# Requesting residual rows one tile earlier, splitting the last product of the second layer, and moving two copies at the layer change

## The reference

```python
# attention: q pooled in pairs, out = softmax(q_pool @ k.T / 8) @ v
x = attn_out.transpose(0, 2, 1, 3).reshape(1152, 512)
# layer m=0: top-1 routing, each expert takes at most cap tokens
e = argmax(x @ w_gate); g = softmax(x @ w_gate)[e]
out[i] = g[i] * (relu(x[i] @ w1[e]) @ w2[e])      # kept tokens, else 0
# layer m=1: tokens with x @ w_skip > 0 are routed without a limit
do = x @ w_skip > 0
out = x.copy()
out[do] = x[do] + g * (relu(x[do] @ w1b[e]) @ w2b[e])
```

## Time and profile before

| | |
|---|---|
| median of 3 runs | 615.25 us (614.92 to 615.62) |
| the profiled execution, its own time | 616.29 us |
| its span, first to last instruction | 614.5 us |
| outside the span | 1.8 us |
| PE busy | 591.7 us (96%) |
| DVE, ACT, POOL busy | 313.5 (51%), 266.3 (43%), 188.5 us (31%) |
| mean granted clock of PE | 0.992 of full speed |

### The profile page before, as it was taken

The page is one execution under the profiler, slowest core; times in us unless marked ns, Lnnn a source line. Parts: engine busy times, 40 slices in busy tenths (PEclk is TensorE's granted clock), DMA queues, the critical chain, the costliest instruction groups (busy, mean ns, idle before and its releaser), DMA issues.

```text
span 614.5 us, 12427 instructions
## 1 busy us (share of the span) xinstructions
PE 591.7 (96%) x3711; PEld 351.9 (57%) x3712; DVE 313.5 (51%) x659; ACT 266.3 (43%) x438; POOL 188.5 (31%) x164
## 2 busy tenths in 40 slices
PE   8899999999999999999999999999899999999992
PEld 7677787777777777777333333333594333333330
DVE  5457565757575766656353963955665220322220
ACT  4655565555565655620344444442102444444410
POOL 4785535444352800001011121122212122222222
PEclk9999999999999999999999999999989999999997
DMA  8979818171621062004999697762757789831111
GB/s 205 291 185 257 185 40 170 43 161 50 145 47 38 3 221 107 22 11 138 402 404 362 256 391 274 260 272 64 272 186 253 265 306 330 318 135 44 45 52 55
DMA packets 42637, 111.61 MB, mean 182 GB/s; under 512 B 16020, under 2 KB 16020, under 8 KB 41536
## 3 DMA queue, kind: packets, MB, share of 16 engines
q1 hardware_dynamic: 38528, 99.03, 50.8%
q0 software_dynamic: 4080, 12.22, 5.7%
HBM read 102.68 MB, written 12.06 MB: 187 GB/s over the span
## 4 chain that ended last, share of the span: by engine, by line
PE 88%; DVE 3%; issue 3%; DMA 2%; ACT 2%; POOLq 0%; DVEq 0%; POOL 0%; SPq 0%; ACTq 0%
PE psum L932 40%; PE psum L701 14%; PE psum L715 12%; PE psum L749 9%; PE psum L919 4%; PE psum L782 3%; PE psum L840 2%; PE psum L761 1%; PE psum L745 1%; DVE probs L1204 1%; ACT probs L1045 1%; PE psum L934 1%; DMA qraw<-in_q_dram 1%; DMA res<-moe_in,idx_r 1%; DMA xraw<-moe_in,rows_in 1%
## 5 line engine op out<-in xcount | busy, mean ns | idle before, releaser
L932 PE MATMUL psum<-w1ring,XT 128*64 x304 | 134.5, 595 | 0.8 <-issue 0.3
L932 PE MATMUL psum<-w2ring,HT 128*64 x320 | 133.7, 571 | 1.3 <-DVE wright L318 0.7
L934 PE MATMUL psum<-wright,XT 128*64 128x512 f32 x304 | 134.5, 595 | 0.0
L934 PE MATMUL psum<-wright,HT 128*64 128x512 f32 (+1 forms) x320 | 133.7, 571 | 0.0
L1204 DVE TENSOR_SCALAR_CACHE_REDUCE probs<-psum 128x1152 f32<-128x1152 f32 x72 | 97.6, 1357 | 62.5 <-PE psum L701 62.5
L1045 ACT ACTIVATE probs<-probs,nmax 128x1152 f32<-128x1152 f32 x72 | 90.7, 1260 | 45.6 <-DVE probs L1204 45.6
L701 PE MATMUL psum<-KT,QT 128*128 128x384 f32 x480 | 102.0, 350 | 2.7 <-DVE probs L1204 1.8
L932 PEld LDWEIGHTS psum<-w2ring,HT 128*64 128x64 f32 x320 | 43.7, 137 | 85.0 <-issue 83.0
L701 PEld LDWEIGHTS psum<-KT,QT 128*128 128x128 f32 x480 | 80.2, 188 | 14.7 <-issue 7.9
L932 PEld LDWEIGHTS psum<-w1ring,XT 128*64 128x64 f32 x304 | 40.1, 137 | 79.7 <-issue 79.7
L715 PE MATMUL psum<-ident,probs 128*128 128x128 f32 x648 | 82.0, 275 | 1.1 <-ACT probs L1045 0.6
(11 more groups left out here) (164 smaller groups left out, 636.7 us busy)
## 6 DMA issues: line engine op xcount, KB each, us to landing
w1ring<-in_moe_w_dram SPq DMA_DIRECT2D x64, 512.0 KB, 7.1
w2ring<-in_moe_w_dram SPq DMA_DIRECT2D x64, 512.0 KB, 7.4
qraw<-in_q_dram SPq DMA_DIRECT2D x30, 288.0 KB, 10.1
kraw<-in_k_dram SPq DMA_DIRECT2D x14, 576.0 KB, 9.0
V<-in_v_dram SPq DMA_DIRECT2D x8, 576.0 KB, 3.9
moe_in<-zero SPq DMA_DIRECT2D x9, 256.0 KB, 3.1
wnext<-in_next_w_dram SPq DMA_DIRECT2D x1, 2304.0 KB, 17.2
out_dram<-moe_in SPq DMA_DIRECT2D x1, 2304.0 KB, 9.4
```

The costliest lines, as they stand in the source:

```text
L932: pe.matmul(psum[0:GRAIN, b, 0:width], lhs[:, c * P:c * P + GRAIN], left, start=first, stop=last, skip_group_check=True)
L934: return pe.matmul(psum[GRAIN:P, b, 0:width], lhs[:, c * P + GRAIN:(c + 1) * P], wright[k][:, cols], start=first, stop=last, skip_group_ch ...
```

## The change

On POOL the order of requests in `step(t)` changes, and in layer 1 the residual rows are those of tile t instead of t-1. Before: residual rows of tile t-1, x of tile t+2, store of y of tile t-1. Now: residual rows of tile t, store of y of tile t-1, x of tile t+2. In layer 0, which has no residual, the store now stands ahead of x. Behind the loop, layer 1 no longer requests residual rows; it waits for a new semaphore `orow_half` and stores.

On PE the last y product of layer 1 also goes through `last_y_product`, in two halves; DVE adds the residual to each half by itself. The two copies of `yT` at the end of layer 0 move from DVE to ACT. DVE's wait with a value from a table becomes a wait for the constant 1 on a semaphore of its own, `last_logits`. PE reads the expert of the first tile ahead of `turn_x(0)` instead of behind it, and `keep_busy` between the counts and `r_ids` issues 13 products instead of 14, in both layers.

```diff
@@ -197,7 +197,8 @@
-        ylast_copied, y_half = sem("ylast_copied"), sem("y_half")
+        ylast_copied, last_logits = sem("ylast_copied"), sem("last_logits")
+        y_half_, orow_half = [sem(f"y_half_{m}") for m in range(2)], sem("orow_half")
...
@@ -633,18 +634,16 @@
                 def count_before(t):
 
                     if isinstance(t, int):
-                        return {0: 0, 1: 0, 2: 1 + m}[t]
-                    return t * (2 + m) - (3 + m)
-
-                def after(t, n):
-                    return count_before(t) + 1 + n
+                        return {0: 0, 1: m, 2: 1 + 2 * m}[t]
+                    return t * (2 + m) - 3
 
                 def step(t, first=False):
-                    if m == 1 and not first:
-                        load_residual(t - 1, after(t, 0))
-                    load_x(t + 2, after(t, 0 if first else m))
+                    count = count_before(t)
+                    if m == 1:
+                        load_residual(t, count + 1)
                     if not first:
-                        store_y(t - 1, after(t, m if isinstance(t, int) else m + 1))
+                        store_y(t - 1, count + (1 + m))
+                    load_x(t + 2, count + (2 + m))
 
                 n = ROUTED[m]
                 token = token_id if m == 0 else slot_token
@@ -667,13 +666,13 @@
                 with pool.Fori(2, NSLOT) as t:
                     with pool.If(t < rest + 2):
                         step(t)
-                done = rest * (2 + m) + (1 + m)
+                done = rest * (2 + m) + (1 + 2 * m)
                 if m == 0:
                     store_y(rest + 1, done + 1, last=True)
                     pool.wait_ge(y_stored, rest * 16 + 32)
                 else:
-                    load_residual(rest + 1, done + 1)
-                    store_y(rest + 1, done + 2)
+                    pool.wait_ge(orow_half, 1)
+                    store_y(rest + 1, done + 1)
                 pool.wait_ge(x_loaded, rest * 16 + 64)
                 settle()
 
@@ -884,7 +883,7 @@
                     for t in range(n):
                         mm = counted(whole, t, t + 1, n + 1)
                 mm.then_inc(pos_ready, 1)
-                keep_busy((14, 14)[m], HID_BANK + 1)
+                keep_busy((13, 13)[m], HID_BANK + 1)
 
                 pe.wait_ge(ids_ready, m + 1)
                 for t in range(n):
@@ -934,10 +933,14 @@
                     return pe.matmul(psum[GRAIN:P, b, 0:width], lhs[:, c * P + GRAIN:(c + 1) * P], wright[k][:, cols],
                                      start=first, stop=last, skip_group_check=True)
 
-                def hidden_product(t):
+                def hidden_place(t):
 
                     expert = left_expert(t)
-                    slot = pe.snap(ring_slot(FIRST, m, expert))
+                    return expert, pe.snap(ring_slot(FIRST, m, expert))
+
+                def hidden_product(t, place=None):
+
+                    expert, slot = place or hidden_place(t)
                     wait(pe, relu_ready, t)
                     for c in range(DC):
                         pe.wait_ge(w_loaded[FIRST][c], expert * 16 + (E * m + 1) * 16)
@@ -980,7 +983,7 @@
                             at = c * DM + half * 2 * P
                             mm = product(SECOND, HT, (Y_BANK, X_BANK)[half], c, slice(at, at + 2 * P), slot,
                                          c == 0, c == FC - 1, 2 * P)
-                        mm.then_inc((y_half, y_done)[half], 1)
+                        mm.then_inc((y_half_[m], y_done)[half], 1)
 
                 def turn_hidden(t):
                     pe.wait_ge(relu_ready, t + 1)
@@ -1007,8 +1010,8 @@
                                        start=(c == 0), stop=(c == DC - 1))
                     mm.then_inc(lg_done, 1)
 
-                def step(t, first=False):
-                    hidden_product(t)
+                def step(t, first=None):
+                    hidden_product(t, first)
                     if first:
                         pe.wait_ge(gates_found, m + 1)
                     else:
@@ -1018,9 +1021,10 @@
 
                 pe.wait_ge(tables_ready, m + 1)
                 rest = pe.value_load(tab_n[m][0:1, 0:1], min_val=0, max_val=NSLOT - 2)
+                own = hidden_place(0)
                 turn_x(0)
                 keep_busy(3, HID_BANK + 1)
-                step(0, first=True)
+                step(0, first=own)
                 step(1)
                 with pe.Fori(0, (NSLOT - 2) // GROUP) as g:
                     with pe.If(g * GROUP < rest):
@@ -1028,10 +1032,8 @@
                             t = pe.snap(g * GROUP + (i + 2))
                             with pe.If(t < rest + 2):
                                 step(t)
-                if m == 1:
-                    y_product(rest + 1)
-                else:
-                    last_y_product(rest + 1)
+                last_y_product(rest + 1)
+                if m == 0:
                     keep_busy(2, HID_BANK + 1)
                     turn_y()
                     keep_busy(2, HID_BANK + 1)
@@ -1185,10 +1187,14 @@
                 relu(rest + 1)
                 copy_hidden(rest + 1)
                 if m == 0:
-                    act.wait_ge(y_half, 1)
+                    act.wait_ge(y_half_[0], 1)
                     nc.scalar.copy(ylast[:, 0:2 * P], bank(Y_BANK, 2 * P)).then_inc(ylast_copied, 1)
                     act.wait_ge(y_done_[0], rest + (2 + START))
                     nc.scalar.copy(ylast[:, 2 * P:4 * P], bank(X_BANK, 2 * P)).then_inc(ylast_copied, 1)
+                    for i in range(2):
+                        half = slice(i * 2 * P, (i + 1) * 2 * P)
+                        act.wait_ge(y_turned, i + 1)
+                        nc.scalar.copy(yT[:, half], bank(YT_BANK + i)[:, half]).then_inc(yt_ready, 1)
 
 
         @block.vector
@@ -1411,7 +1417,7 @@
 
                 L = logits[:] if m == 0 else logits2[:, :, 0:E]
                 if m == 1:
-                    dve.wait_ge(lg_copied, dve.value_load(tab_n[0][:], min_val=0, max_val=NSLOT - 2) + 2)
+                    dve.wait_ge(last_logits, 1)
                     nc.vector.tensor_scalar(active[:], logits2[:, :, E], 0.0, 2.0 * E, ALU.is_gt, ALU.mult).then_inc(active_ready, 1)
 
                 reduce(of(r_max), L, ALU.max)
@@ -1518,16 +1524,18 @@
                     with dve.If(t < rest + 1):
                         step(t)
                 if m == 0:
-                    for i in range(2):
-                        half = slice(i * 2 * P, (i + 1) * 2 * P)
-                        dve.wait_ge(y_turned, i + 1)
-                        nc.vector.tensor_copy(yT[:, half], bank(YT_BANK + i)[:, half]).then_inc(yt_ready, 1)
                     at = bass.ds(rest + 1, 1)
                     dve.wait_ge(lg_done, 1)
                     nc.vector.tensor_copy(logits2[:, at, :].rearrange("p o c -> p (o c)"), bank(LG_BANK, E + 1)
-                                          ).then_inc(lg_copied, 1)
+                                          ).then_inc(last_logits, 1)
                 else:
-                    copy_y(m, rest + 1)
+                    dve.wait_ge(y_stored_[1], rest * 16 + 16)
+                    dve.wait_ge(res_loaded, rest * 16 + 32)
+                    dve.wait_ge(y_half_[1], 1)
+                    nc.vector.tensor_tensor(orow[:, 0:2 * P], bank(Y_BANK, 2 * P), res[:, 0:2 * P], ALU.add).then_inc(orow_half, 1)
+                    dve.wait_ge(y_done_[1], rest + (2 + START))
+                    nc.vector.tensor_tensor(orow[:, 2 * P:4 * P], bank(X_BANK, 2 * P), res[:, 2 * P:4 * P], ALU.add
+                                            ).then_inc(y_copied_[1], 1)
 
 
 _INS = ["q", "k", "v", "moe_w_gate", "moe_w1", "moe_w2", "moe2_w_skip", "moe2_w_gate", "moe2_w1", "moe2_w2"]
```

## The result

The changed kernel takes 610.60 us (median of 4 runs, 609.67 to 611.32) against 615.43 us (4 runs of the kernel before, 614.92 to 616.12). The ratio is 0.9922, with a 95% interval of 0.9910 to 0.9933: 4.8 us faster, where 6.8 us were forecast (608.45 us, range 607.1 to 610.8). Measured once more with more rounds, 6 runs gave 610.32 us and a ratio of 0.9913 (0.9898 to 0.9928).

A forecast was written before the change was run, and what follows sets the result against it. PE bounds layer 1's tiles, leaving gains in the tail (hung on POOL's queue), the change of layers and the routings. Terms 3.7 + 2.8 + 0.2 + 0.1 = 6.8 us; 615.25 - 6.8 = 608.45 us, range 607.1 to 610.8.

The forecast's parts named there:

- The tail, 3.7 us: End of layer 1: the last store begins at 605.3 instead of 608.99, a gain of 3.7 us.
- The change of layers, 2.8 us: Between layer 0 and layer 1: three gains of 1.5, 0.5 and 0.8 us, together 2.8 us.
- (a): Between the layers: with the `yT` copies on ACT, the logits are copied at 445.5, a gain of 1.5 us.
- (b): Between the layers: DVE's 0.59 us idle behind the logits copy falls under 0.1, a gain of 0.5 us.
- (c): Layer 1's counts: if the clock stays at 2.4 GHz, PE's waiting products end in time, a gain of 0.8 us.
- keep_busy, 0.2 us: Ahead of `r_ids`: one product less lets PE begin 0.2 us earlier in layer 0, nothing in layer 1.
- The expert read ahead, 0.1 us: Around the first tile's transposes of x: reading the expert earlier gains 0.1 us for both layers, between -0.2 and 0.8.
- x in last place, 0: Layer 1's tiles: x, requested third, lands after 6.9 us with 1.2 us of slack; nothing counted.
- The second case: Rival, between the layers: the clock falls all the same, gain 5.7 us, 609.5 us; chance 13 in 100.
- The other rivals: Layer 1: x late, 609.7 us (9 in 100); x much later, no faster (5); tail less, 610.3 (9); only middle, 612.2 (4).
- POOL's rounds: Tail rival: POOL's rounds take 2 us more, so the tail gains only 1.9 us, 610.3 us; chance 9 in 100.

The follow-up runs named there:

- the tail alone: Kernel before plus only POOL's new request order, no residual gather behind the loop, and layer 1's last y product in halves: 611.71 us, ratio 0.9946.
- the change of layers alone: Kernel before plus only the `yT` copies on ACT and DVE's wait for a constant on `last_logits`: 612.92 us, ratio 0.9953.

## Why the prediction was right, and where its size was off

**Right in direction, in range, and in its mechanisms.** The sum was 6.8 us, the span gained 6.5. The time gained 4.8 to 5.1.

- *The tail, 3.7 us.* 4.04 us between the two first profiled executions (12.56 to 8.52), 3.7 in the median of the tail alone. The second profile of before has 12.16, as its residual gather landed in 4.0 us and not in 4.4. The store was put 8.9 us behind the first matmul of the last y product; it was 8.52 to 8.67. PE's chain was worked out at 8.52 and is that. POOL's came sooner than worked out: its first request follows DVE's addition by 1.50 us (592.47 to 593.97), not by 1.85. So both chains end within 0.2 us of each other, and that POOL's is the later holds in the kernel with the tail alone, not in the full one. The term took the split at no cost. It wins 0.43 us in the span and costs about 0.5 us outside (2.7 in the middle against 2.19).
- *The change of layers, 2.8 us.* (a) 1.5 us: 1.33 (4.08 to 2.75). (b) 0.5 us: 0.56 (0.59 to 0.03). (c) 0.8 us for the clock: 0.7 to 1.15 in an execution in which it falls. The whole: 2.89 between the profiled executions (20.49 to 17.60), 2.8 with this part alone.
- *keep_busy, 0.2 us.* It is in the trace and lost in the gather's scatter of 0.5 us. In layer 1 nothing, as said: POOL's product is what PE waits for. *The expert read ahead, 0.1 us.* Not seen.
- *x in last place, 0.* Right: issued 4.42 us after the first request (4.43 forecast), landed after 6.6 us (6.9), 1.8 us of slack (1.2).

**The step that failed** is one sentence: "so the median after is 615.25 - 6.8 = 608.45 us". It carried the whole difference of one profiled execution over to the median. But 0.8 us of it was a half clock that comes, by the clocks, in about half of the executions, and its residual gather took longest to land of the six profiles with the old tail (4.4 us, against 3.6 to 4.2). So the execution was 1.04 us above the median. The median span of before is 613.55, 0.95 us under the profiled one. And the sum took the time outside the span as constant, 1.8 us; it became about 2.7.

Between the two profiled executions the sum missed little. The tail gave 0.3 us more than its term and the change of layers 0.1, ACT's moved code took 0.3, and the start of layer 0 came 0.2 us later (287.34 against 287.14) where 0.3 were counted as gained; with 0.1 us in the tiles of layer 0, that is 6.5. The medians of the spans differ by 5.75 (613.55 to 607.8), as the profiled execution of before stood 0.95 above its median and that of the changed kernel 0.2. Less the 0.95 outside, 4.8 us are left, and 4.8 to 5.1 were measured.

The parts do not add up, either: 3.7 for the tail and 2.8 for the change of layers, each alone, are 6.5 us of median span, and both with the small edits make 5.75. The tail of the kernel with the change of layers alone is already short, 11.43 us (594.06 to 605.49) instead of 12.16 to 12.56, as ACT's moved code lets PE begin its last y product 0.3 us later while the end hangs on POOL, and the residual gather landed in 3.6 us. From there to 8.52 only 2.9 us are left for the tail's part. Why that gather landed sooner in this kernel and in the one with two more copies on ACT, no run shows.

The second case, that the clock falls all the same, did not happen in either profile, and all 10 executions of the changed kernel have 0.994 to 0.998. The other rivals fell too: PE never waits for x in the tiles, and POOL's rounds ran as before. The chances of the listed cases add up to 0.95 for faster and 0.02 for the same, where 0.93 and 0.04 stand.

**What is shown of the code's position, and what is open.** The Trainium skill (Runtime: NRT & Kernel Launch, Instruction fetch mechanics) says that an engine's code is fetched in blocks while it runs, and that the step from one block to the next is mostly hidden. The traces agree that loads go on while the kernel runs, and show two places where they are not hidden: behind the last instruction, where the time outside the span grows with the end of the last packet, and at ACT's copy, where a packet 0.65 to 0.83 us after the copy's start goes with 0.3 us of delay. That the load causes this delay is argued from all 14 profiles, and not tested otherwise. DVE's 0.39 us with the memsets look like the same thing, as the q14 packet that stood behind the last instruction now stands 0.8 to 0.9 us after the start of its last addition (602.54 and 603.32); this is argued as well. That the q8 packet is PE's is likely, as it stands near the end in two of the three profiled executions with the split, which lengthens PE's code, and in no other. The Trainium skill (Runtime: NRT & Kernel Launch, Terms) also names sequences that the runtime puts around a kernel, with resets of semaphores. The three new semaphores are not what adds the 0.4 us: six memsets took them away and left the semaphores.

## What to carry to other kernels

A sum of differences from one profiled execution is a forecast of that execution. Look first at how the runs differ among themselves, by span and clock, and count a term that comes only in a part of them by that part. When a wait goes that ended last, work out the next chain to the same point as well; here the two stood some 0.15 us apart, and the split, which shortened PE's alone, won 0.43 us in the span and nothing in time. Under half a microsecond, an edit's effect cannot be told from what it does to the place of the code behind it, unless a kernel with unread instructions stands beside it, or the packets of the instruction queues are looked up, also behind the last instruction. And of two parts that both end on the same wait, each alone may show a gain that the two together do not.

## What the runs showed of the hardware

- Two unread one-column copies on ACT, 150 us ahead, made ACT's wake for a copy 0.3 us later (0.71 to 1.01 us after PE's transposes begin); six took the delay away, and moved the q14 instruction packet near it from 592.95 to 581.36 us.
- The time outside the span depends on a kernel's code: 1.71 to 1.83 us in 29 executions; 2.15 to 2.21 with DVE's code shorter by some rows, with one q14 packet behind the last instruction; back to 1.72 to 1.81 with six memsets on DVE, without that packet; up to 3.07 with the split, where one profile shows a 16 KB q8 packet that ends 3.3 us behind the last instruction.
- A granted half clock between the layers stands in four of five profiles in which PE is idle there for 1.36 to 1.60 us, not in the one with 1.60, and in none of nine in which that idle time is filled or removed. It costs 0.7 to 1.15 us.
